# Attention and two mixers in one kernel: q is transposed by VectorE in 32x32 blocks, and the k-v product moves in front of the q product

## What is computed

```
kv  = einsum('bhsd,bhse->bhde', k, v)            # b = h = 8, s = 576, d = 64
o   = einsum('bhsd,bhde->bhse', q, kv)
x   = o / sqrt(mean(o*o, -1) + 1e-6) * g_norm    # then heads side by side: [8, 576, 512]
u   = x + (x.T @ U @ V).T                        # low rank, 32
x2  = u + relu(u @ w_ch1) @ w_ch2                # 512 -> 2048 -> 512
h   = gelu_tanh(x2 @ w_in); u2, v2 = halves of h
out = x2 + (u2 * (w_sg @ layernorm(v2)*g_ln + b_sg)) @ w_out
```

## Time and profile before

| | us |
|---|---|
| median of 3 runs | 1367.31 |
| lowest, highest | 1367.31, 1832.47 |
| the profiled execution | 1368.81 |
| its span, first to last instruction | 1367.0 |
| first attention unit to first up step | 8 to 46 |
| up tile 0, with units 4 to 7 | 46 to 126 |
| a later up tile | 65 |

### The profile page before, as it was taken

One profiled execution on the slowest core, in us unless ns is written; L12 is line 12 of the kernel. 1 busy time (PEld: TensorE's weight loads), 2 busy tenths in 40 slices (PEclk: granted clock), 3 DMA queues, 4 the chain that ended last, 5 costly groups with the idle time before them and its releaser, 6 DMA issues.

```text
span 1367.0 us, 22208 instructions
## 1 busy us (share of the span) xinstructions
PE 1307.4 (96%) x8590; PEld 1254.3 (92%) x8590; DVE 868.1 (64%) x1228; ACT 541.6 (40%) x892; POOL 97.9 (7%) x107
## 2 busy tenths in 40 slices
PE   5799999999999998999999999999999999999998
PEld 5688999999999988989999999998898998998987
DVE  4977575656565758888888888885642624425322
ACT  4554434444343432455444454535222322223221
POOL 6220000000000000000000000000210210111100
PEclk9999999999999999999999999999999999999999
DMA  9444445454545426736537174441012021120211
GB/s 233 126 139 130 148 132 155 131 165 149 163 131 158 131 96 217 274 124 221 173 104 257 55 271 146 162 154 60 19 60 79 10 77 39 49 77 23 66 39 39
DMA packets 182023, 170.27 MB, mean 125 GB/s; under 512 B 94112, under 2 KB 152496, under 8 KB 181952
## 3 DMA queue, kind: packets, MB, share of 16 engines
q1 hardware_dynamic: 178992, 164.42, 38.1%
q0 software_dynamic: 1600, 4.56, 1.2%
q10 hardware_dynamic: 1360, 0.30, 0.1%
HBM read 101.08 MB, written 66.06 MB: 122 GB/s over the span
## 4 chain that ended last, share of the span: by engine, by line
PE 83%; DVE 8%; ACT 3%; issue 2%; DMA 2%; SPq 1%; POOL 0%; DVEq 0%; ACTq 0%; POOLq 0%
PE ps L1366 24%; PE ps L1368 24%; PE ps L1367 24%; PE ps L1371 3%; PE ps L1395 2%; PE ps L1387 2%; PE ps L1403 1%; DVE w L1008 1%; DMA hT_scratch<-h_st 1%; DVE x_lo L1035 1%; DVE h_st L1059 1%; PE ps L1614 1%; PE ps L1615 1%; DVE y L975 1%; ACT w L702 1%
## 5 line engine op out<-in xcount | busy, mean ns | idle before, releaser
L1366 PE MATMUL ps<-x_hi,w 128*128 128x288 f32 x896 | 273.6, 305 | 26.4 <-DVE h_st L1059 7.5
L1367 PE MATMUL ps<-x_lo,w 128*128 128x288 f32 x896 | 266.3, 297 | 0.0
L1368 PE MATMUL ps<-x_hi,w 128*128 128x288 f32 x896 | 265.9, 297 | 0.0
L1366 PE MATMUL ps<-r_hi,w_hi 128*128 128x384 f32 x672 | 225.0, 335 | 3.0 <-DVE r_lo L1187 1.9
L1368 PE MATMUL ps<-r_hi,w_lo 128*128 128x384 f32 x672 | 224.5, 334 | 0.0
L1367 PE MATMUL ps<-r_lo,w_hi 128*128 128x384 f32 x672 | 224.5, 334 | 0.0
L827 ACT ACTIVATE r_hi<-hb 128x768 fp32r<-128x768 f32 x168 | 142.2, 848 | 169.3 <-PE ps L1368 164.3
L1366 PEld LDWEIGHTS ps<-x_hi,w 128*128 128x128 f32 x896 | 170.1, 190 | 31.8 <-DVE h_st L1061 7.9
L1367 PEld LDWEIGHTS ps<-x_lo,w 128*128 128x128 f32 x896 | 170.5, 190 | 0.0
L1368 PEld LDWEIGHTS ps<-x_hi,w 128*128 128x128 f32 x896 | 170.5, 190 | 0.0
L1329 DVE SCALAR_TENSOR_TENSOR vs<-ps,glcol,bias_bc 128x576 f32<-128x576 f32 x32 | 26.1, 815 | 199.8 <-PE ps L1615 199.5
(11 more groups left out here) (166 smaller groups left out, 2494.9 us busy)
## 6 DMA issues: line engine op xcount, KB each, us to landing
hT_scratch<-h_st SPq DMA_DIRECT2D x64, 576.0 KB, 4.7
hb<-hT_scratch SPq DMA_DIRECT2D x24, 1536.0 KB, 7.2
uT_scratch<-x_raw SPq DMA_DIRECT2D x32, 288.0 KB, 2.3
x_st<-uT_scratch SPq DMA_DIRECT2D x24, 384.0 KB, 3.5
x2T_scratch<-x_st SPq DMA_DIRECT2D x24, 384.0 KB, 6.8
x_raw<-x2T_scratch SPq DMA_DIRECT2D x8, 1152.0 KB, 6.0
k_raw<-in_k SPq DMA_DIRECT2D x64, 128.0 KB, 3.0
v_raw<-in_v SPq DMA_DIRECT2D x32, 256.0 KB, 3.0
```

The costliest lines, as they stand in the source:

```text
L1366: mm(dst, ws[0], xs[0], start=first, stop=False)
L1367: mm(dst, ws[0], xs[1], start=False, stop=False)
L1368: return mm(dst, ws[1], xs[0], start=False, stop=last)
```

## The change

q is loaded by four transfers per unit instead of three, each with 32 features of all 576 tokens, as 128-byte pieces onto 32 partitions: partition j of a block holds tokens j, j+32, ... with 32 features each. One VectorE instruction transposes all 32x32 blocks of 128x576 into `qT`. TensorE's transposes of q and ScalarE's two copies go. The transpose stands at at_ 6 of the unit before (behind the low part of y, and behind the add of idx 2 in a tile's first unit), at the start ahead of `sums`. The k-v product of the next unit moves from at_ 2 to at_ 0, directly in front of the attention product, and its copy by ScalarE from at_ 4 to at_ 1, ahead of `std`. In SyncE's program k and v are issued before q. Tokens of U, V, b_sg, w_sg and the output are in natural order; k and v keep the old one.

```
+        def q_block(slot, i):
+            return q_raw[slot][QB * i:QB * (i + 1), :].rearrange("p (b i) -> p b i", i=QB)
+        def q_block_source(b, a, i):
+            return rows(q, b)[:, 2 * a + i // 2, :, QB * (i % 2):QB * (i % 2 + 1)].rearrange("o (b j) i -> j (o b) i", j=QB)
...
             def load_q(b, a, m, slot):
                 if m > HP:
-                    sp.wait_ge(s_qt, 2 * m)
+                    sp.wait_ge(s_qsb, m)
...
-                for h in range(2):
-                    sp.dma_start(q_raw[slot][:, 0:JM, h, :], x[:, h, 0:SM, :].rearrange("o (p j) d -> p (o j) d", j=JM)).then_inc(s_q[m % HP], 16)
-                sp.dma_start(q_raw[slot][0:ST, JM, :, :], x[:, :, SM:S, :].rearrange("o h p d -> p (o h) d")).then_inc(s_q[m % HP], 16)
+                for i in range(4):
+                    sp.dma_start(q_block(slot, i), q_block_source(b, a, i)).then_inc(s_q[m % HP], 16)
             def load_next(n):
                 if n < B * HP:
+                    load_kv(n // HP, n % HP, n, 0)
                     load_q(n // HP, n % HP, n, 0)
-                    load_kv(n // HP, n % HP, n, 0)
...
-            def q_copy(m, bx, first=False):
-            def q_copy_tail(m, by):
...
                     if at_ == 0:
                         attn_copy(m, BX, BY)
                         squares(m, sq)
-                    elif at_ == QK:
+                    elif at_ == 1 and more:
+                        kv_copy(m + 1, BY, P)
+                    elif at_ == 2:
                         std(m)
-                        if more:
-                            q_copy(m + 1, BX)
-                    elif at_ == QK + 1:
+                    elif at_ == 3:
                         y_high(m)
-                    elif at_ == QK + 2 and more:
-                        act.wait_ge(s_kv, m + 2)
-                        q_copy_tail(m + 1, BY)
-                        kv_copy(m + 1, BY, P)
...
+            def q_transposed(m, slot, times):
+                dve.wait_ge(s_q[slot], 64 * times)
+                if not (isinstance(m, int) and m == 0):
+                    dve.wait_ge(s_out, 2 * m)
+                raw = q_raw[slot] if isinstance(m, int) and m < HP else q_raw[0]
+                nc.vector.transpose(qT[:].rearrange("p j m -> p (j m)")[:, 0:S], raw[:]).then_inc(s_qsb, 1)
...
             for m in range(HP):
                 ym = y_first[m % 3]
+                kv_copy(m + 1, 2)
+                q_transposed(m + 1, (m + 1) % HP, (m + 1) // HP + 1)
                 sums(m, sq_first)
-                kv_copy(m + 1, 2)
                 normalise(m, ym)
...
                 if at_ == 0:
                     pe.wait_ge(s_uev, m)
+                    if more:
+                        pe.wait_ge(s_kvsb, 2 * (m + 1))
+                        k_v(m + 1, BY, (r + 1) % HP, t + 2 + (r + 1) // HP, P)
                     attention(m, BX, BY)
-                elif at_ == QK and more:
-                    pe.wait_ge(s_o, 2 * (m + 1))
-                    q_transposed(m + 1, BX, BY, (r + 1) % HP, t + 2 + (r + 1) // HP)
-                    k_v(m + 1, BY, (r + 1) % HP, t + 2 + (r + 1) // HP, P)
```

More of the change, by code:

```diff
@@ L23 @@
 NCP = 2 * NJ - 1
+QB = 32
 VB = (0, NJ, NCP)
@@ L36 @@
 NX = NI + 2
-PERIOD, QK, LOW, UT = 12, 2, 8, 11
+PERIOD, LOW, UT = 12, 8, 11
 LAST_UT = (HP - 1) * PERIOD + UT
@@ L117, in build @@
     v_raw = at("v_raw", [P, 2, NJ, HD], F32)
-    q_raw = at("q_raw", [P, NJ, 2, HD], F32)
+    q_raw = at("q_raw", [P, S], F32)
     qT = at("qT", [P, NJ, P], F32)
@@ L145, in build @@
     cursor[0] = h_st_off
-    q_raw = [q_raw] + [at(f"q_raw{i}", [P, NJ, 2, HD], F32) for i in range(1, HP)]
+    q_raw = [q_raw] + [at(f"q_raw{i}", [P, S], F32) for i in range(1, HP)]
     y_first = [y] + [at(f"y{i}", [P, NJ, P], F32) for i in range(1, 3)]
@@ L562, in _ @@
             sp.wait_ge(s_wsT, NJ + 1)
-            sp.wait_ge(s_bb, 2)
+            sp.wait_ge(s_bb, 1)
             store_out(0, 0)
@@ L650, in bank @@
                 return ps[:, n, a:b]
-            def q_copy(m, bx, first=False):
[L653 to L656, removed]
-            def q_copy_tail(m, by):
-                act.wait_ge(s_qt, 2 * m + 2)
-                nc.scalar.activation(qT[:, JM, :], bank(by, 0, P), ACT.Copy).then_inc(s_qsb, 1)
             def kv_copy(m, bx, at_=0):
@@ L727, in x2_high @@
                 nc.scalar.activation(x2_hi[par][:, :, 0:n], x2_raw[par][:, :, 0:n], ACT.Copy).then_inc(s_x2hi, 1)
[L730 to L733, removed]
+            for i in range(4):
+                act.dma_start(q_block(0, i), q_block_source(0, 0, i)).then_inc(s_q[0], 16)
             for n in range(2):
                 act.dma_start(gcol[HD * n:HD * (n + 1), :], g_norm.rearrange("(p o) -> p o", o=1)).then_inc(s_g, 16)
-            act.wait_ge(s_zero, 3 * HP + 6)
-            q_copy(0, 0, first=True)
-            q_copy_tail(0, 1)
+            act.wait_ge(s_zero, 2 * HP + 7)
             for m in range(HP):
@@ L1111, in up_tile @@
                         y_low(m)
+                    elif at_ == 6 and (r + 1 < HP or not end):
+                        q_transposed(m + 1, (r + 1) % HP, t + 2 + (r + 1) // HP)
                     elif at_ == LOW:
@@ L1371, in transpose @@
                 return mm(dst, src, identF[:], is_transpose=True, start=start, stop=stop)
-            def q_transposed(m, bx, by, slot, times):
-                pe.wait_ge(s_q[slot], 48 * times)
-                raw = q_raw[slot] if isinstance(m, int) and m < HP else q_raw[0]
-                for j in range(JM):
-                    ins = transpose(ps[:, bx, j * P:(j + 1) * P], raw[:, j], True, True)
-                ins.then_inc(s_qt, 1)
-                transpose(ps[:, by, 0:P], raw[:, JM], True, True).then_inc(s_qt, 1)
             def k_v(m, bx, slot, times, at_=0):
@@ L1431, in _ @@
                     u_transposed(m - 2, 4, y_first[m - 2])
-                q_k_v_first(m + 1)
+                k_v_first(m + 1)
                 if m == 1:
-                    pe.wait_ge(s_low, 3)
+                    pe.wait_ge(s_low, 2)
                 if m:
@@ L1450, in attention_step @@
                     pe.wait_ge(s_uev, m)
+                    if more:
+                        pe.wait_ge(s_kvsb, 2 * (m + 1))
+                        k_v(m + 1, BY, (r + 1) % HP, t + 2 + (r + 1) // HP, P)
                     attention(m, BX, BY)
-                elif at_ == QK and more:
-                    pe.wait_ge(s_o, 2 * (m + 1))
-                    q_transposed(m + 1, BX, BY, (r + 1) % HP, t + 2 + (r + 1) // HP)
-                    k_v(m + 1, BY, (r + 1) % HP, t + 2 + (r + 1) // HP, P)
                 elif at_ == LOW:
-                    if more:
-                        pe.wait_ge(s_qsb, 2 * (m + 1) + 1)
                     low_rank(m, BX)
@@ L1575, in w_sg_transposed @@
                 for t in range(NJ):
-                    src = ws_raw[:, t, j:SM:JM] if j < JM else ws_raw[:, t, SM + (NJ - j) * ST:SM + (NJ - j) * ST + P]
+                    src = ws_raw[:, t, j * P:(j + 1) * P] if j < JM else ws_raw[:, t, SM + (NJ - j) * ST:SM + (NJ - j) * ST + P]
                     ins = transpose(ws_tile(j, NJ * P)[:, t * P:(t + 1) * P], src, True, True)
```

49 lines of the change are left out of this document (18 added, 31 removed).

## The result

The changed kernel takes 1384.42 us (median of four runs, 1381.11 to 1385.77) against 1367.31 before: 1.0122 times as long, with a 95% interval of 1.0097 to 1.0146. That is 17.1 us slower, within 2%. One of the four runs of the kernel before took 1832.47 us and is left out of the comparison as a slow one. The forecast was 1373.5 us (1366 to 1380 by its own sum, 1352 to 1384 with parts of the rivals); the median lies 0.4 us above the upper end.

What follows compares the result with a forecast made beforehand. TensorE is busiest (62.9 of 65 us), but places where VectorE's chain is already later decide. Start 2.9, rest of first tile 2, steady 1.3: +6.2 on 1368.8 gives 1375.0, median 1.5 lower: 1373.5 us (1366 to 1380; with rivals 1352 to 1384).

Steps and rivals of the forecast that it cites:

- Part 1: Up tiles: removing five PE transposes and two q copies frees 0.55 us of TensorE per unit, 15.4 us if nothing becomes late.
- Part 2: Steady up tiles: k-v product before attention shortens cover; +0.3 us per tile, +1.3 us for the steady part instead of -15.4.
- cover: TensorE work between attention and the steps needing the chain's results; forecast 1.6 us less of it per unit.
- The wait at step 8: Sign: once per steady tile, matmuls wait 1.2 us at step 8 for the add of idx 2, not seen before.
- Part 3: VectorE's q transpose takes 0.75 us, hidden at step 6 of steady units; at the start it stands ahead of sums.
- up steps start 2.0 us later: Start: two transposes, 1.5 us, and the k-v copy ahead of sums delay the first up step by 2.0 us.
- Part 4: Queues: TensorE waits 3.6 us for unit 5's v; step 3 of the first tile +2.9 us; steady loads cost nothing.
- Rest of tile 0: First up tile after step 3, where VectorE also splits w1: taken as +2 us (-1 to +4).
- C: Rival, chance 0.12: start and first tile 5 to 15 us worse through lower TensorE clock and GpSimd's w1 sums; 1384 us.
- A: Rival, chance 0.22: the cover holds in steady tiles and only the start costs; 1354.8 us, tiles of 62.5 us.
- B: Rival, chance 0.06: VectorE held at the transpose by q's landing or its own length; 1414 us at 3 us of hold.
- part 5: Natural token order: fewer, unstrided copies of V and bias, some 0.5 us at the start beside a data wait; counted as nothing.

Runs made afterwards that it cites:

- e3: Changed kernel with the k-v product back behind step 2 and ScalarE's kv copy back at step 4, VectorE's transpose kept: 1362.0 us, 0.9952 of the kernel before.
- e11: Kernel before with the k-v product in front of attention, k and v issued ahead of q from unit 5 on: 1382.2 us, ratio 1.0085.
- e2: Changed kernel with, at the start, VectorE's kv copy behind sums and its transpose behind normalise: 1380.6 us, 1.0081 of the kernel before.
- e4: Changed kernel with only ScalarE's kv copy moved from step 1 to behind y_high (step 4): 1380.7 us, 1.0085 of the kernel before.
- e5: Changed kernel with GpSimd's last eight w1 transfers (2 MB) held until unit 4's q has landed: 1381.3 us, 1.0102 of the kernel before.
- e6: Changed kernel with unit 5's loads issued before the third store of u instead of behind the fourth: 1383.0 us, 1.0109 of the kernel before.
- e8: Changed kernel with the edits of e3 and e2 together, loads and stores in the changed kernel's order: 1360.0 us, 0.9929 of the kernel before.
- e9: e8 with GpSimd's last w1 transfers also held until unit 4's q has landed: 1360.0 us, 0.9935 of the kernel before.
- e10: e3 with VectorE transposing each q of the up tiles' units twice, one behind the other: 1361.4 us, 0.9947 of the kernel before.
- e7: Changed kernel with the four edits of e2, e3, e5 and e6 together: 1364.9 us, 0.9978 of the kernel before.
- e1b: Kernel before with each large q transfer cut in two by partitions, five transfers per unit, pieces still 256 bytes: 1375.9 us, ratio 1.0047.

## Why the prediction was right in direction and short in size

**Part 1** (five transposes are 0.55 us of TensorE) held to 0.02 us: e3 wins 0.53 to 0.56 us per unit.

**Part 2** (cover) was walked as +0.75, -0.55, -0.55 and +0.67 us for the four units; tile 4 shows +0.72, -0.54, -0.55 and +0.77. (4.40 + 2.25 in the first unit is 6.65, not 6.70; it changes nothing.) The wait at step 8 is there, 1.01 us of idle and the step 1.17 us longer; that at step 44 grew to 1.42 us with 0.48 more two steps earlier. One line of the walk was too dark, without effect here: the 0.2 us of slack in the first unit was not all, since y_high also stood behind the copy of an up product. e3 took 0.55 us of cover away and nothing waited. Tiles 1 to 6 are 2.2 us longer against 1.3; 0.8 of that is in tile 2 alone, where the others have 0.4 and less, and why is open.

**Part 3**: the transpose takes 0.771 us on average; I had 0.75. The 0.66 us worked out from the Trainium skill (VectorE: DVE Perf Modes, The TRN2 errata) is 0.11 too low here; the same section says that this row comes out too low for single operations. Hidden in steady units, as said. The step that failed is the start: "up steps start 2.0 us later (0.7 to 4)". It was 6.1 us in this profile and 4 to 8 over the four profiles with this start. I counted the two transposes' own 1.5 us and took q for landed; VectorE waited for it. The line's group (32 transposes) has 11.1 us of waiting for q, all before 42 us. 7.3 of them are the wait for the very first q, when there is nothing else to do; the other 3.8 are 1.85 us for unit 2's q, 0.27 for unit 3's and 1.63 for unit 4's:

```profile
L1056 DVE STREAM_TRANSPOSE qT<-q_raw 128x576 f32<-128x576 f32 x32 | 24.7, 771 | 11.1 <-DMA q_raw<-in_q 11.1
```

**Part 4**: "issue at 50.0, product at 52.9" was wrong by the start: the last piece was issued at 54.84, the product ran at 57.57. The wait itself, 3.6 us forecast, was 3.91. "DMA has room" was shown for a steady tile (share 0.48) and used for the start, where the share was 0.78 to 1.10. Counting the issues would have told a third of it: nine per unit instead of eight, so four more of 0.63 us, 2.5 us, stand ahead of the end of unit 4's q, the last load issued at the start. It moved by 7.9 us, from 26.0 to 33.9, across the issue of GpSimd's 2 MB of w1 (28.64 us before, 31.21 now), because issues took longer too: four of q 2.6 to 3.9 us instead of 2.5, one of k 2.21 instead of 0.63. Why they did is open; they fall where the DMA share is 1.1 to 1.2.

**Rest of tile 0**, taken as +2, is the largest miss: tile 0 is 9.2 us longer against 2.9. By steps: step 0 is 6.3 us longer (3.9 waiting, the k-v product, and both products at the lower clock), step 2 is 3.3 shorter. In steps 27 to 31, behind GpSimd's sums and VectorE's split of w1 side by side (L990 took 3.03 us there, 2.42 beside GpSimd near 70 us, 2.02 to 2.03 otherwise), 4.6 us are lost, 2.0 by a longer wait and 2.6 at 1.44 us a step instead of 0.80, with the granted clock at 0.54 on average from 91.5 to 95.2 us. The remaining 1.5 us are smaller differences. e11 has none of the changes at the start, starts at 45.0 us, and has the same 88.2 us: so the start and the q loads are not needed for this loss, and the k-v product's place, with the order of loads that e11 shares, is enough. With the product in front and the changed start tile 0 takes 83.7 to 87.9 us (changed, e2, e4, e5, e6), with the product at step 2 it takes 77.9 to 79.7 (e3, e8, e9, e10; e7 apart), so 4 to 10 us are its price, in single profiles.

**Rivals.** C, "start and first tile worse through the clock and GpSimd's w1 sums", at 1384 us with a chance of 0.12, hits the number: 1384.4. That is half luck. The span missed the forecast by 10.7 us, and only tile 0's 6.3 of them have C's mechanism, which is in the rows: clock 0.50 in 45 to 60 us, VectorE beside GpSimd. The start's 4.1 come from q's late landing, which C does not have. A needed the cover to hold; it holds once the product stands at step 2, and e3 is A in the steady tiles (62.64 us) with the loss of the start. B, VectorE held at the transpose, did not come in the tiles (no transpose there waits for q, and e10's 1.55 us of hold cost nothing), but it is the right picture of unit 3 at the start.

**The rest of part 4 and part 5.** e3 wins 2.2 us per steady tile, which is four times the 0.55 us of the transposes, so the 128-byte pieces and the new order of tokens cost nothing there that shows.

Open: why one and the same start differs by 4 us between profiles, and how much of tile 0's loss is the clock alone; no run held the clock still.

## What to carry to other kernels

A matmul moved in front of a chain can cost up to its own time where another engine's chain ends last (here 0.76 and 0.24 of 1.1 us, and nothing in the other two units), while the matmuls removed elsewhere win nothing there; so count the cover per unit before moving work ahead of the product that starts the chain. Price added transfers in the stage where the DMA engines are busiest, by their number and by what another queue issues next to them, not in the steady stage. When a change is a package, run its parts in a table of two by two: here the one part (VectorE's transpose) is a gain of 0.5% and the other hid it.

## What the runs showed of the hardware that I had not expected

Splitting transfers at equal bytes and pieces cost 7.2 us (e1b); in its profile the last of them was issued beside 2 MB of another queue and landed 11.2 us after its issue, against 5.0 us for the same load in the kernel before. With those 2 MB held back on the changed kernel (e5) it was 4.9 us instead of 8.3. Halving the pieces from 256 to 128 bytes at an equal number of transfers added only 1.2 us. VectorE's operations of 128x512 took up to 1.78 us beside GpSimd's on the same kind of operand (e7), and 0.69 us alone.
